# Common table set, direct first tiles, fillers; the one-hot low columns made by three comparisons of 1536 elements with repeated operands

## The reference

```python
# attention: batch 4, 8 heads, 576 positions, head size 64, window of 64 keys
scores = scale * np.matmul(q, k.transpose(0, 1, 3, 2))
mask = (rel >= 0) & (rel < window)
scores = np.where(mask, scores, -1e9)
attn = softmax(scores)
x = (attn @ v) reshaped to 2304 tokens x 512
# routing: two of eight experts for each token
noisy_logits = x @ w_gate + np.log1p(np.exp(x @ w_noise)) * noise
top2 = indices of the two largest; top2_w = softmax over the two
# experts
for e in range(8):
    for k in range(2):
        mask = top2[:, k] == e
        h = np.maximum(x[mask] @ w1[e], 0.0)          # 512 -> 1024
        out[mask] += top2_w[mask, k, None] * (h @ w2[e])   # 1024 -> 512
# dense layer, 512 -> 2048 -> 512
h = x @ w_in
g = np.where(h >= 1, h, np.where(h <= -1, 0.0, (h + 1) ** 2 / 4))
return g @ w_out
```

## Time and profile before

| | |
|---|---|
| median of 3 runs | 1114.3 us (1113.38 to 1115.14) |
| the profiled execution | 1113.99 us, of which the span is 1112.3 |
| PE busy | 1074.6 us, 97% of the span |
| DVE, ACT, POOL busy | 349.9, 347.5, 355.2 us |
| mean granted clock of PE | 0.98; under full mainly at 111 to 167 us |
| transfers | 121.97 MB, mean 110 GB/s |

### The profile page before, as it was taken

One profiled execution on the slowest core, in us unless ns is written; L12 is line 12 of the kernel. 1 busy time (PEld: TensorE's weight loads), 2 busy tenths in 40 slices (PEclk: granted clock), 3 DMA queues, 4 the chain that ended last, 5 costly groups with the idle time before them and its releaser, 6 DMA issues.

```text
span 1112.3 us, 19443 instructions
## 1 busy us (share of the span) xinstructions
PE 1074.6 (97%) x6597; PEld 930.4 (84%) x6598; DVE 349.9 (31%) x685; ACT 347.5 (31%) x796; POOL 355.2 (32%) x230
## 2 busy tenths in 40 slices
PE   8999388999999999999999999999999999999998
PEld 6999256888888888888888887989989899899997
DVE  5888630221122122112211221434224142241321
ACT  4666211222122212212221221514325243252441
POOL 3000068559462809073543604930110100101000
PEclk8999769999999999999999999999999999999999
DMA  9785455995441424333332401320210201102000
GB/s 244 219 231 156 133 166 203 352 321 176 150 164 45 141 85 132 113 113 114 99 146 75 162 27 58 123 57 1 57 47 9 57 8 48 47 9 57 9 11 19
DMA packets 68707, 121.97 MB, mean 110 GB/s; under 512 B 25728, under 2 KB 30976, under 8 KB 68160
## 3 DMA queue, kind: packets, MB, share of 16 engines
q0 software_dynamic: 16688, 62.66, 17.0%
q1 hardware_dynamic: 38496, 34.72, 10.8%
q10 hardware_dynamic: 13488, 24.12, 6.7%
HBM read 87.66 MB, written 33.82 MB: 109 GB/s over the span
## 4 chain that ended last, share of the span: by engine, by line
PE 89%; POOL 4%; issue 3%; DMA 2%; DVE 0%; SPq 0%; ACT 0%; ACTq 0%; POOLq 0%; DVEq 0%
PE bank L1064 7%; PE bank L1066 7%; PE bank L1065 7%; PE bank L1049 7%; PE bank L1051 7%; PE bank L1050 7%; PE bank L1126 6%; PE bank L1127 6%; PE bank L1128 6%; PE bank L1113 6%; PE bank L1112 6%; PE bank L1111 6%; PE bank L1072 3%; PE bank L937 3%; POOL Wl L387 2%
## 5 line engine op out<-in xcount | busy, mean ns | idle before, releaser
L387 POOL TENSOR_TENSOR Wl<-stage,Wh 128x2048 fp32r<-128x2048 f32 x36 | 165.8, 4605 | 3.0
L1111 PE MATMUL bank<-zT_h,Wh 128*128 128x256 f32 x576 | 163.1, 283 | 1.0 <-DVE zT_l L874 1.0
L1113 PE MATMUL bank<-zT_h,Wl 128*128 128x256 f32 x576 | 163.1, 283 | 0.0
L1112 PE MATMUL bank<-zT_l,Wh 128*128 128x256 f32 x576 | 163.1, 283 | 0.0
L840 DVE COPY y_out<-bank 128x512 f32<-128x512 f32 x43 | 29.7, 692 | 368.6 <-PE bank L1066 368.6
L1049 PE MATMUL bank<-Wh,xT_h 128*128 x344 | 140.1, 407 | 5.2 <-DVE xT_l L831 4.5
L1051 PE MATMUL bank<-Wh,xT_l 128*128 x344 | 136.0, 395 | 0.0
L1050 PE MATMUL bank<-Wl,xT_h 128*128 x344 | 135.6, 394 | 0.0
L1064 PE MATMUL bank<-Wh,hT_h 128*128 x344 | 134.1, 390 | 0.2
L1066 PE MATMUL bank<-Wh,hT_l 128*128 x344 | 134.2, 390 | 0.0
L1065 PE MATMUL bank<-Wl,hT_h 128*128 x344 | 133.8, 389 | 0.0
(11 more groups left out here) (156 smaller groups left out, 1657.5 us busy)
## 6 DMA issues: line engine op xcount, KB each, us to landing
stage<-w POOLq DMA_DIRECT2D x32, 1024.0 KB, 5.5
y_sorted<-y_out ACTq DMA_DIRECT2D x43, 256.0 KB, 2.1
x_in<-x_sorted ACTq DMA_DIRECT2D x41, 256.0 KB, 2.7
x_sorted<-gath_a SPq DMA_DIRECT2D x23, 256.0 KB, 4.5
x_sorted<-gath_b SPq DMA_DIRECT2D x20, 256.0 KB, 5.3
x_rows<-x_blk SPq DMA_DIRECT2D x36, 128.0 KB, 3.4
out<-o_out SPq DMA_DIRECT2D x36, 128.0 KB, 2.2
q_bd<-qT SPq DMA_DIRECT2D x16, 256.0 KB, 4.5
```

The source lines that it names most:

```text
L387: nc.gpsimd.tensor_tensor(Wl[:, s, cols], stage[:, c % 2], Wh[:, s, cols], ALU.subtract).then_inc(w_ready, 1)
L1111: nc.tensor.matmul(here, high, zT_h[:, k], start=(k == 0), stop=False)
L1112: nc.tensor.matmul(here, high, zT_l[:, k], start=False, stop=False)
L1113: mm = nc.tensor.matmul(here, low, zT_h[:, k], start=False, stop=(k == KD - 1))
```

## The change

Four things change. ACT loads one table set that holds both the exponential and the logarithm, at its start ahead of its transfers. The first 4 tiles (DIRECT), not 2, are read from the gather buffers; SP bounces tiles from 4 on, ACT fetches from 4 on, and POOL issues 8 gathers, not 6, before `first_parts`. PE gets fillers: 28 before the rank sums, 28 before the one-hot products, 16 instead of 12 before the tiles, and 6 behind the transposes of each of tiles 0 and 1. And `oh_lo` is made by 3 comparisons of two tensors, 1536 elements each, instead of 36 comparisons of 128 elements with a scalar; its low parts are bf16 now (`lo_b`).

```diff
-    GB, LAG = 8, 2
+    GB, LAG, DIRECT = 8, 2, 4
...
-            for t in range(LAG):
-                bounce(t, t, 16)
-            LOOPED = (TILES - LAG) // GB
+            for t in range(DIRECT, DIRECT + LAG):
+                bounce(t, t % GB, 16 * (t // GB) + 16)
+            LOOPED = (TILES - DIRECT - LAG) // GB
             with sp.Fori(0, LOOPED) as m:
-                for r in range(GB):
-                    at = (r + LAG) % GB
-                    bounce(GB * m + r + LAG, at, 16 * m + (16 if r + LAG < GB else 32))
-                    confirm(r, 16 * m + 16)
+                for k in range(DIRECT, DIRECT + GB):
+                    bounce(GB * m + k + LAG, (k + LAG) % GB, 16 * m + 16 * ((k + LAG) // GB) + 16)
+                    confirm(k % GB, 16 * m + 16 * ((k - DIRECT) // GB) + 16)
...
-                if t == 6:
+                if t == GB:
                     first_parts(1, 1, 1)
-                if t == 12:
+                if t == GB + 4:
                     last_parts(1, 1)
                     fetch_first(2)
-                if t >= GB:
-                    pool.wait_ge(bounced_r[t % GB], 16 * (t // GB))
-                if GB <= t < GB + 2:
+                if GB <= t < GB + DIRECT:
                     pool.wait_ge(xg_done, t - GB + 1)
+                elif t >= GB + DIRECT:
+                    pool.wait_ge(bounced_r[t % GB], 16 * ((t - DIRECT) // GB))
...
+            nc.scalar.preload_act_table_set("natural_log_exp_and_others")
...
-                act.wait_ge(bounced, t + 1)
+                act.wait_ge(bounced, t - DIRECT + 1)
...
             for u in range(2):
                 high_x(u, u)
-            for u in range(2):
-                fetch(2 + u, u)
             act.wait_ge(y_cleared, 16 * (TILES - SURE))
...
-            then(nc.vector.tensor_copy(lo_f[:], slot_lo[:]))
+            then(nc.vector.tensor_copy(lo_b[:], slot_lo[:]))
...
-            for c in range(2 * NT):
-                inst = nc.vector.tensor_scalar(oh_lo[:, c], io_lo[:], lo_col[:, c:c + 1], None, ALU.is_equal)
-                if c % PART == PART - 1:
-                    inst.then_inc(onehots, 1)
+            for c in range(0, 2 * NT, PART):
+                nc.vector.tensor_tensor(oh_lo[:, c:c + PART], io_lo[:].unsqueeze(1).to_broadcast([P, PART, P]),
+                                        lo_col[:, c:c + PART].unsqueeze(2).to_broadcast([P, PART, P]),
+                                        ALU.is_equal).then_inc(onehots, 1)
...
             pe.wait_ge(zeroed, 5)
+            keep_busy(banks[4], 28)
             pe.wait_ge(route, ROUTE_PICKED)
...
             mm.then_inc(rank_done, 1)
+            keep_busy(banks[4], 28)
...
-            keep_busy(banks[4], 12)
+            keep_busy(banks[4], 16)
             pe.wait_ge(tables_ready, 1)
             def x_rows_of(t, u):
-                return x_in[:, u] if has(t, 2) else gath(u)
+                return x_in[:, u] if has(t, DIRECT) else gath(t)
...
-                    transpose_x(t + 2, u, 16 * m + 16)
-            transpose_x(0, 0, 0)
-            transpose_x(1, 1, 0)
+                    transpose_x(t + 2, u, 16 * m)
+            for t in range(2):
+                transpose_x(t, t, 0)
+                keep_busy(banks[4], 6)
```

More of the change, by code:

```diff
@@ L159, in build @@
             hi_b = sb("hi_b", [P, 2, NT], BF16)
-            lo_f = sb("lo_f", [P, 2, NT])
+            lo_b = sb("lo_b", [P, 2, NT], BF16)
             oh_rank = sb("oh_rank", [P, 2, NT, E])
@@ L312, in confirm @@
                 sp.sem_inc(bounced, 1)
-            for t in range(LAG):
-                bounce(t, t, 16)
-            LOOPED = (TILES - LAG) // GB
+            for t in range(DIRECT, DIRECT + LAG):
+                bounce(t, t % GB, 16 * (t // GB) + 16)
+            LOOPED = (TILES - DIRECT - LAG) // GB
             with sp.Fori(0, LOOPED) as m:
-                for r in range(GB):
-                    at = (r + LAG) % GB
-                    bounce(GB * m + r + LAG, at, 16 * m + (16 if r + LAG < GB else 32))
-                    confirm(r, 16 * m + 16)
[L322 to L326, removed]
+                for k in range(DIRECT, DIRECT + GB):
+                    bounce(GB * m + k + LAG, (k + LAG) % GB, 16 * m + 16 * ((k + LAG) // GB) + 16)
+                    confirm(k % GB, 16 * m + 16 * ((k - DIRECT) // GB) + 16)
+            for t in range(DIRECT + GB * LOOPED, TILES):
+                if t + LAG < TILES:
+                    bounce(t + LAG, (t + LAG) % GB, 16 * ((t + LAG) // GB) + 16)
+                confirm(t % GB, 16 * ((t - DIRECT) // GB) + 16)
             def keep(u, count):
@@ L798, in _ @@
             hi_row, t_row = (a[:].rearrange(pairs).unsqueeze(1) for a in (hi_b, io_t))
-            lo_col = lo_f[:].rearrange(pairs)
+            lo_col = lo_b[:].rearrange(pairs)
             then(nc.vector.tensor_tensor(oh_hi[:], all_hi[:], hi_row.to_broadcast([P, TILES, 2 * NT]), ALU.is_equal))
@@ L1016, in _ @@
             mm.then_inc(ids_done, 1)
-            keep_busy(banks[4], 12)
+            keep_busy(banks[4], 16)
             pe.wait_ge(tables_ready, 1)
             def x_rows_of(t, u):
-                return x_in[:, u] if has(t, 2) else gath(u)
+                return x_in[:, u] if has(t, DIRECT) else gath(t)
             def transpose_x(t, u, k):
-                if has(t, 2):
+                if has(t, DIRECT):
                     pe.wait_ge(x_fetched[u], k)
```

## The result

| | median, us | lowest to highest | runs |
|---|---|---|---|
| before | 1114.3 | 1110.55 to 1115.29 | 7 |
| changed | 1106.65 | 1104.05 to 1109.84 | 7 |

The ratio is 0.9937 with a 95% interval of 0.9919 to 0.9955: 5 to 9 us faster. Forecast was 1104.1, in a range of 1100.5 to 1108.5. The profiled execution took 1104.05 us (span 1102.5), 9.9 less than the profiled one of before; it is the fastest of the seven. Its mean granted clock was 0.994, that of the six others 0.987 to 0.991.

The account below looks back on a forecast made before the run. PE was taken to set the pace, busy 97% of the span, with gains to be won before 188 us. Terms 1.3 + 0.65 + 0.8 - 0.8 - 0.3 + 2.4 + 4.6 + 1.6 = 10.25 gave 1104.1 us, range 1100.5 to 1108.5.

Parts of the forecast that it names:

- table load: ACT's load between exponential and logarithm in the routing goes, and DVE waits there for nothing else: gain 1.3 us.
- rank products: The 18 rank products on PE take 0.7 us at full clock instead of 1.37: gain 0.65.
- comparisons and one-hot products: Three comparisons of 1.76 us replace 36 taking 5.94; read-out follows the last by 2.24 as before: gain 0.8.
- fillers behind them: 16 fillers after the one-hot products, 11 at low clock, take 5.7 us against 4.88: loss 0.8.
- first transposes to H of tile 0: Fillers between the first tiles stand mostly in PE's waits, before the read of the weight slot: loss 0.3 us.
- H of tile 0: With fillers keeping PE's clock, it takes 5.59 us as in tile 1, not 8.01: gain 2.4.
- the stall: From Y of tile 0 to the next H, 11.31 us becomes 6.68 as ACT stops waiting for SP: gain 4.6.
- the low clock behind it: The low clock of 184 to 187 us followed the stall; H there took 7.20 against 5.59: gain 1.6.
- Half-stall rival: Idleness before the loop's first H is PE's loop entry and stays: 3.6 us less gain, 1107.7; chance 0.18.
- The fillers before the rank sums: 28 fillers at 0.21 us take 5.9, cover PE's wait and end in time if the clock stays up.
- fourth rival: Fillers run at 1.2 GHz, 0.42 us each, and outlast PE's waits: 4.1 us slower, 1118.4; chance 0.03.
- full-clock rival: Clock is full at the end of the one-hot products: 0.85 and 1.4 us more gain, 1101.9; chance 0.15.

Follow-up runs that it names:

- direct_only: The kernel before with the four direct tiles alone, nothing else of the change: 1107.31 us, ratio 0.9948.
- nofill_contiguous: The changed kernel with the fillers of before and the low columns compared in a layout without the repeated last dimension: 1103.4 us, ratio 0.9908.
- again: The changed kernel itself, unchanged, run and profiled a second time: 1106.04 us, ratio 0.9927 to the kernel before.
- two_direct: The changed kernel with only tiles 0 and 1 direct and SP, POOL and ACT ordered as before: 1114.3 us, ratio 0.9984.
- pace: The changed kernel with its second 28 fillers replaced by 24 products reading with an 18-element step, then 24 contiguous: 0.155 against 0.04 us per product.
- sized_contiguous: The changed kernel with fewer fillers (16, 20, 10, the sixes) and the contiguous comparisons: 1101.97 us, ratio 0.9900.

## Why the forecast was right, and where it was off

Start to start in the two profiled executions, gains in us (forecast in brackets); together they make the 9.8 between the spans:

| part | gain |
|---|---|
| attention, up to DVE's first routing step (121.50, 122.16) | -0.66 (0) |
| table load | 1.28 (1.3) |
| rank products | 0.64 (0.65) |
| comparisons and one-hot products | 0.32 (0.8) |
| fillers behind them | -0.31 (-0.8) |
| first transposes to H of tile 0 (4.79, 4.18) | 0.61 (-0.3) |
| H of tile 0 | 2.43 (2.4) |
| from there to Y of tile 0 | 0.10 (0) |
| the stall (11.31, 6.68) | 4.63 (4.6) |
| the low clock behind it | 1.63 (1.6) |
| the rest, 923 us | -0.84 (0) |

- **The table load, the stall and its clock**: right in mechanism and size. Half-stall rival: fell, no gap before the loop's first H remains. The stall's end is shown by `direct_only` as well; that its low clock of 1.6 comes in every execution is not. The load moved to the start costs nothing: ACT's first transfer is issued at 1.01 us, beside the load.
- **H of tile 0**: the 2.4 came out in these two profiles, and that is in part luck. The term took the 8.01 us of one execution for what the kernel always does and put the whole gain down to the fillers. With the direct tiles and no fillers there H took 5.57 and 5.56 in two profiles (`direct_only`, `nofill_contiguous`) and 7.20 and 7.17 in two others: in such a kernel the sixes gain 0 to 1.6, by the execution. How often the kernel before has the stretch, one profile cannot tell.
- **The fillers before the rank sums**: this step failed. It said that they end in time "if the clock stays up, and it was up where they start". That was one execution. Of the five profiles with these 28 fillers the clock held in three and fell at or shortly before their start in two, `again` (2.0 us late) and `two_direct` (8.80 us of fillers, 1.7 late). It is the fourth rival, which had a chance of 0.03 and was to decide "once a filler takes more than 0.24 us": in `again` the mean is 0.32. In the six other executions of the changed kernel the mean clock was 0.987 to 0.991 against 0.994, so they had more time at the low clock; where, is not known. Forecast for all filler terms together was a gain of 1.95; leaving the added ones out costs nothing that the times show (0.9921 against 0.9927, each to 0.0013 or 0.0017). That is the likeliest part of the difference between 10.2 forecast and 7.7 measured; how the 2.5 divide over the terms is not shown.
- **The comparisons**: each is as priced, the gain is not. The term counted the time to the last comparison and added before's 2.24. But from the first product to the read-out it is 6.09 us before and 6.04 after: the products set the time already, and what was won is the start of the first of them, 2.09 us behind the first comparison before and 1.81 after. The 0.85 of the full-clock rival would not have come either: the clock was full for nearly half of the products and they were no faster.
- **The fillers behind the products**: 0.3 lost, not 0.8. The clock came back 3.5 us after their start (143.66 to 147.2) and not 4.6, so more of the 16 ran at the full one.
- **The time from the first transposes to H**: 4.15 to 4.29 in every profile with four direct tiles, fillers or not, and 4.79 and 5.02 with two (`before`, `two_direct`). So these 0.6 come with the direct tiles; by which way was not tried.
- **The rest**: two of the first eight steps from Y to Y took 12.55 and 12.82 us instead of 12.25 (before: 12.47 and 12.36), and the last 8.63 instead of 8.34. In all fourteen profiles the rest lies between 922.3 and 923.7 us (before 922.6, after 923.4), so this is no more than what executions differ by; the cause of the longer steps is open.
- **The start**: the routing starts at 120.24 to 124.24 us, with or without the table load at the start, and at 123.10 and 123.91 in versions that do not differ from the changed kernel there. The 0.66 is scatter and no cost that the runs show.

The two profiled executions differ by 9.8 us, close to the 10.25 of the sum, but they are one of each kernel: after was the fastest of seven, with the clock held in the first fillers, and before had the low stretch in H of tile 0, which may not come each time. The medians, 7.7 apart, are the better measure.

## What to carry to other kernels

Size a group of fillers by the low clock and not by the full one: here it must fit its wait at 0.42 us each, or it holds back the work behind it in the executions in which the clock has fallen. Before pricing a low stretch of the clock, look whether it comes in a second execution of the same code: here the one in the first tile did not always. A stall that hangs on another engine's queue (here a confirmation behind a gather behind weight pieces) can take back part of what is won ahead of it (0.9 of 2.9 us in `two_direct`), so it goes first. Before making a producer faster, take the consumer's rate from its own rows: here the products stood at 0.16 us each at either clock, and the run `pace` points at the step of their moving operand. And compare two profiles from a common event, not from the start of the span, which here was off by up to 4 us.

## What was not expected of the hardware

- A product that reads 86 bf16 columns with a step of 18 elements takes 0.155 us against 0.04 contiguously, both at the full clock; with a step of 36 it is 0.16 at the full and at the low clock.
- Weights read with a step of 12 elements (`nofill_contiguous`): a load of 146 ns (median) against 128, and 36 products in 6.05 us against 5.93 (6.03 in `sized_contiguous`).
- The same program meets PE's clock in different places in different executions: mean clock of 0.987 to 0.994 and times of 1104.05 to 1109.84 in seven executions of the changed kernel.
